# Softmax row sums divided out after the attention product instead of before it, and the q/k load issued in the middle of a pair

## What is computed

```python
def _attn_ref(q, k, v, proj):          # q, k, v: (2, 8, 768, 64); proj: (64, 6)
    q_bits = (einsum('bhsd,dk->bhsk', q, proj) > 0); k_bits = the same of k
    mask = q_bucket[:, :, :, None] == k_bucket[:, :, None, :]     # bucket: the 6 bits as a number
    scores = np.where(mask, scale * (q @ k.T), -1e9)
    scores = scores - max(scores, axis=-1)
    attn = np.exp(scores)
    attn = attn / (np.sum(attn, axis=-1, keepdims=True) + 1e-09)
    return attn @ v                                              # then x: (1536, 512)
def _moe_ref(x):  return ((x @ w1) * (x @ w2)) @ w3 @ w_out      # 512 -> 1024 -> 512
def _moe2_ref(x): return (sigmoid(x @ w_gate) * (x @ w_val)) @ w_out   # 512 -> 1536 -> 512
```

## Time and profile before

| | |
|---|---|
| three runs | 819.89, 815.14, 820.67 us |
| span of the profiled execution, first to last instruction | 813.6 us |
| TensorE busy | 780.8 us (96%) |
| VectorE busy | 385.2 us (47%) |
| ScalarE busy | 381.8 us (47%) |
| GpSimd busy | 232.3 us (29%) |
| attention stage, from the first pair's step 1 to the first MLP matmul | 21.62 to 315.92 us |

### The profile page before, as it was taken

One profiled execution on the slowest core, in us unless ns is written; L12 is line 12 of the kernel. 1 busy time (PEld: TensorE's weight loads), 2 busy tenths in 40 slices (PEclk: granted clock), 3 DMA queues, 4 the chain that ended last, 5 costly groups with the idle time before them and its releaser, 6 DMA issues.

```text
span 813.6 us, 11907 instructions
## 1 busy us (share of the span) xinstructions
PE 780.8 (96%) x3992; PEld 675.8 (83%) x3992; DVE 385.2 (47%) x888; ACT 381.8 (47%) x678; POOL 232.3 (29%) x146
## 2 busy tenths in 40 slices
PE   6799999999799998999999999999999999999998
PEld 4677887879597887999999888888888888888886
DVE  5799999999999996422222111111111111121220
ACT  5688888888688896323322121222313312221211
POOL 3767365462627332211211121113212312100000
PEclk9999999999999999999999999999999999999999
DMA  6662534537343400100000002002202010000101
GB/s 157 195 168 64 148 84 123 123 94 169 77 113 99 118 28 27 52 27 27 26 0 0 1 27 77 27 2 77 77 1 77 14 63 26 0 26 27 39 26 39
DMA packets 22055, 51.68 MB, mean 64 GB/s; under 512 B 3304, under 2 KB 5992, under 8 KB 22032
## 3 DMA queue, kind: packets, MB, share of 16 engines
q1 hardware_dynamic: 21808, 51.32, 22.5%
q10 hardware_dynamic: 224, 0.07, 0.0%
HBM read 29.43 MB, written 3.15 MB: 40 GB/s over the span
## 4 chain that ended last, share of the span: by engine, by line
PE 80%; DVE 7%; SPq 5%; DMA 5%; issue 2%; ACT 1%; DVEq 0%; ACTq 0%
PE pair_bank L930 14%; PE pair_bank L929 14%; PE pair_bank L928 14%; PE bank L930 6%; PE bank L929 6%; PE bank L928 6%; PE bank L853 5%; PE pair_bank L826 5%; DMA qk_raw<-in_qk 5%; PE bank L838 5%; SPq L218 3%; DVE rowmax L648 2%; DVE pt_lo L681 2%; DVE prob L673 2%; SPq L223 1%
## 5 line engine op out<-in xcount | busy, mean ns | idle before, releaser
L360 POOL TENSOR_TENSOR w_lo<-w_raw,w_hi 128x1024 fp32r<-128x1024 f32 (+1 forms) x36 | 69.5, 1931 | 194.1 <-ACT w_hi L445 192.8
L929 PE MATMUL pair_bank<-x_lo,w_hi 128*128 128x512 f32 (+1 forms) x320 | 117.4, 367 | 0.0
L928 PE MATMUL pair_bank<-x_hi,w_hi 128*128 128x512 f32 (+1 forms) x320 | 117.4, 367 | 0.0
L930 PE MATMUL pair_bank<-x_hi,w_lo 128*128 128x512 f32 (+1 forms) x320 | 117.4, 367 | 0.0
L445 ACT ACTIVATE pt_hi<-bank 128x384 fp32r<-128x384 f32 x192 | 84.9, 489 | 39.3 <-PE bank L838 38.7
L681 DVE TENSOR_TENSOR pt_lo<-bank,pt_hi 128x384 fp32r<-128x384 f32 x192 | 97.6, 549 | 11.7 <-ACT pt_hi L445 11.3
L838 PE MATMUL bank<-ident,prob 128*128 128x128 f32 x576 | 83.5, 280 | 15.8 <-DVE pt_lo L681 14.0
L463 ACT ACTIVATE prob<-pair_bank,ebias,escale 128x768 f32<-128x768 f32 x96 | 95.3, 992 | 5.0 <-DVE ebias L659 5.0
L838 PEld LDWEIGHTS bank<-ident,prob 128*128 128x128 f32 x576 | 67.1, 142 | 35.5 <-DVE pt_lo L681 12.8
L648 DVE TENSOR_REDUCE rowmax<-pair_bank 128x1 f32<-128x768 f32 x96 | 91.2, 950 | 4.3 <-PE pair_bank L826 3.5
L826 PE MATMUL pair_bank<-mk,sq 128*128 128x384 f32 x384 | 89.6, 356 | 1.9 <-ACT prob L463 1.9
(11 more groups left out here) (104 smaller groups left out, 1332.3 us busy)
## 6 DMA issues: line engine op xcount, KB each, us to landing
sq<-hl SPq DMA_DIRECT2D x45, 192.0 KB
w_raw<-in_w SPq DMA_DIRECT2D x32, 256.0 KB, 2.7
mk<-hl SPq DMA_DIRECT2D x15, 384.0 KB
qk_raw<-in_qk SPq DMA_DIRECT2D x7, 768.0 KB, 4.3
wo_raw<-in_wo SPq DMA_DIRECT2D x10, 512.0 KB, 4.1
v_raw<-in_v SPq DMA_DIRECT2D x16, 192.0 KB, 3.4
w_raw<-in_wg SPq DMA_DIRECT2D x12, 256.0 KB, 3.3
w_raw<-in_wv SPq DMA_DIRECT2D x12, 256.0 KB, 3.6
```

The costliest lines, as they stand in the source:

```text
L360: pool.tensor_tensor(dst, src, hi, ALU.subtract).then_inc(w_ready[j], 1)
L928: pe.matmul(dst, hi, m_hi, start=start, stop=False)
L929: pe.matmul(dst, hi, m_lo, start=False, stop=False)
L930: return pe.matmul(dst, lo, m_hi, start=False, stop=stop)
```

## The change

`prob` stays unscaled, and nothing lies any more between the exponential and its transposition. The attention output is multiplied by 1/sum after the two halves of `pv_bank` have been added. There the query rows lie along the free axis, so the reciprocals, which VectorE has as a column of 128 partitions by 3, must be laid along a row and repeated on 64 partitions. That is done by two DMAs a unit, `spread_norm`: one writes the 384 values as single 4-byte elements to a row in DRAM, SP waits until they have landed, and the second reads the row back into 64 partitions of `norm_all`. `attention_sum` on GpSimd becomes two operations, an addition and a multiplication that waits for `norm_all`. Epsilon and reciprocal are taken once a unit. `q_codes` is scaled by ScalarE at step 4 and no longer by GpSimd. SP's q/k load of pair p + 2 is issued in the middle of pair p, in front of the head-0 assembly, where before the load of pair p + 1 stood at the start of pair p.

```diff
-NORM_ON_ACT = (2,)
...
+        norm_row = nc.dram_tensor("norm_row", (4, HALF), F32, kind="Internal").ap()
+        x_own = [at(f"x_own{j}", [128, HALF], F32, a + j * 1536) for j in range(2)]; a += 3 * KB
+        norm_all = [at(f"norm_all{j}", [128, HALF], F32, a + j * 1536) for j in range(2)]; a += 3 * KB
...
-            def pair(p, first=False):
-
-                if not first:
-                    load_qk(p + 1, p + 1, 2 * p + 2)
+            def spread_norm(p, u):
+
+                hd, hf = u // 2, u % 2
+                normed, before, after, kept = (4 * p + u + 1, 16 * p, 16 * p + 16, 2 * p - 1 + hf)
...
+                sp.wait_ge(rnorm_done, normed)
+                at_least(sp, norm_loaded[u], before)
+                sp.dma_start(norm_row[u, :].rearrange("(t p) -> p t", p=128),
+                             rnorm[:, UQ * u:UQ * u + UQ],
+                             allow_slow_non_contiguous=True).then_inc(row_loaded[u], 16)
+                sp.wait_ge(row_loaded[u], after)
+                at_least(sp, x_done, kept)
+                sp.dma_start(norm_all[hf][D * hd:D * hd + D, :],
+                             norm_row[u, :].partition_broadcast(D)).then_inc(norm_loaded[u], 16)
+
+            def pair(p, last=False):
+
                 load_w3(p + 1, 0, p + 1)
                 load_v(p + 1, 0, p + 1)
+                spread_norm(p, 0)
+                if not last:
+                    load_qk(p + 2, p + 2, 2 * p + 4)
                 assemble(0, p + 2, STEPS * p + QT)
+                spread_norm(p, 1)
                 load_w3(p + 1, 1, p + 1)
                 load_v(p + 1, 1, p + 1)
+                spread_norm(p, 2)
                 assemble(1, p + 2, STEPS * p + STEPS)
+                spread_norm(p, 3)
...
             load_mlp(w1_d, w2_d, 0, 0, U1)
             load_mlp(w1_d, w2_d, 1, 1, U1)
+            for u in range(4):
+                spread_norm(PAIRS - 1, u)
...
             def attention_sum(p, hf):
 
                 pool.wait_ge(x_kept, 4 * p - 1 + hf)
+                pool.tensor_tensor(x_tmp[hf][:, :], x_tmp[hf][:, :], x_own[hf][:, :], ALU.add).then_inc(x_added, 1)
+                pool.wait_ge(norm_loaded[hf], 16 * p)
+                pool.wait_ge(norm_loaded[2 + hf], 16 * p)
+                pool.wait_ge(x_added, 2 * p - 1 + hf)
                 pool.tensor_tensor(x_f[:, bass.ds(p - 1, 1), HALF * hf:HALF * hf + HALF],
-                                   x_f[:, bass.ds(p - 1, 1), HALF * hf:HALF * hf + HALF],
                                    x_tmp[hf][:, :].rearrange("p (t n) -> p t n", t=1),
-                                   ALU.add).then_inc(x_done, 1)
+                                   norm_all[hf][:, :].rearrange("p (t n) -> p t n", t=1),
+                                   ALU.mult).then_inc(x_done, 1)
...
-                        scale_q_codes(p + 1)
...
+            def scale_q_codes(p):
+
+                act.wait_ge(codes_done, 2 * (p + 1))
+                act.activation(q_codes, codes[0:2 * CODES, :], ACT.Copy, scale=PEN).then_inc(q_codes_done, 1)
...
-                    if k % UQ in NORM_ON_ACT:
-                        act.wait_ge(rnorm_done, s + 1)
-                        act.activation(prob[k % 3][:, :], prob[k % 3][:, :], ACT.Copy,
-                                       scale=rnorm[:, k:k + 1]).then_inc(norm_done[k % UQ], 1)
...
+                    if k == 4 and not last:
+                        scale_q_codes(p + 1)
...
-            def normalise(p, k):
-                dve.wait_ge(rnorm_done, STEPS * p + k + 1)
-                dve.tensor_scalar(prob[k % 3][:, :], prob[k % 3][:, :], rnorm[:, k:k + 1], None,
-                                  ALU.mult).then_inc(norm_done[k % UQ], 1)
+            def inverse(p, u):
+                dve.wait_ge(eps_done, 4 * p + u + 1)
+                at_least(dve, row_loaded[u], 16 * p)
+                cols = slice(UQ * u, UQ * u + UQ)
+                dve.reciprocal(rnorm[:, cols], rowsum_eps[:, cols]).then_inc(rnorm_done, 1)
...
+                dve.tensor_tensor(out, own, x_tmp[hf][rows, :], ALU.add).then_inc(x_added, 1)
+                dve.wait_ge(x_added, added)
+                dve.wait_ge(norm_loaded[hf], 16 * PAIRS)
+                dve.wait_ge(norm_loaded[2 + hf], 16 * PAIRS)
+                dve.tensor_tensor(out, out, norm_all[hf][rows, :], ALU.mult).then_inc(x_done, 1)
...
-                pe.wait_ge(norm_done[k % UQ], 4 * p + k // UQ + 1)
+                pe.wait_ge(exp_done, s + 1)
```

More of the change, by code:

```diff
@@ L153, in build @@
         exp_done, eps_done, rnorm_done = sem("exp_done"), sem("eps_done"), sem("rnorm_done")
-        norm_done = [sem(f"norm_done{j}") for j in range(UQ)]
+        row_loaded = [sem(f"row_loaded{u}") for u in range(4)]
+        norm_loaded = [sem(f"norm_loaded{u}") for u in range(4)]
+        x_added = sem("x_added")
         t_done, pt_hi_done, pt_lo_done = sem("t_done"), sem("pt_hi_done"), sem("pt_lo_done")
@@ L196, in load_qk @@
             def load_qk(p, split, projected):
+                if not isinstance(projected, int):
+                    sp.compute_val(split)
+                    sp.compute_val(projected)
                 at_least(sp, hl_ready, split)
@@ L227, in assemble_q_codes @@
                 cq = CODES * hd
-                sp.dma_start(sq[hd][D:D + CODES, 1, :].bitcast(F32), q_codes[cq:cq + CODES, :]).then_inc(assembled[hd], 16)
+                sp.dma_start(sq[hd][D:D + CODES, 1, :].bitcast(F32), codes[64 + cq:64 + cq + CODES, :]).then_inc(assembled[hd], 16)
             def assemble(hd, pairs, scored):
@@ L274, in _ @@
             load_v(0, 1, 0)
-            pair(0, first=True)
-            with sp.Fori(1, PAIRS - 1) as p:
+            pair(0)
+            with sp.Fori(1, PAIRS - 2) as p:
                 pair(p)
+            pair(PAIRS - 2, last=True)
             load_mlp(w1_d, w2_d, 0, 0, U1)
             load_mlp(w1_d, w2_d, 1, 1, U1)
+            for u in range(4):
+                spread_norm(PAIRS - 1, u)
             with sp.Fori(1, KF // 2) as i:
@@ L307, in rounded @@
                 return pool.tensor_tensor(dst, src, zero.broadcast_to(list(src.shape)), ALU.add)
[L309 to L314, removed]
             def qk_split(p):
@@ L533, in _ @@
             act.activation(sq[0][D:D + CODES, 1, :], codes[0:CODES, :], ACT.Copy, scale=PEN).then_inc(first_parts, 1)
-            act.activation(q_codes[:, :], codes[0:2 * CODES, :], ACT.Copy, scale=PEN).then_inc(q_codes_done, 1)
+            scale_q_codes(0)
             exp(0, 0)
@@ L682, in transposed_lo, with attention_out @@
                                       pt_hi[(k // UQ) % 2][cut].bitcast(F32), ALU.subtract).then_inc(pt_lo_done, 1)
-            def attention_out(rows, hf, src):
+            def attention_out(rows, hf, own, added):
                 cols = slice(HALF * hf, HALF * hf + HALF)
-                dve.tensor_tensor(x_f[rows, PAIRS - 1, cols], src, x_tmp[hf][rows, :], ALU.add).then_inc(x_done, 1)
+                out = x_f[rows, PAIRS - 1, cols]
+                dve.tensor_tensor(out, own, x_tmp[hf][rows, :], ALU.add).then_inc(x_added, 1)
[3 more added lines that the diff above has]
+                dve.tensor_tensor(out, out, norm_all[hf][rows, :], ALU.mult).then_inc(x_done, 1)
             def code_half(p, hf, src=fill_bank):
@@ L705, in pair @@
                         row_max(*nxt)
-                    sum_eps(p, k)
-                    if nxt:
                         exp_scale(*nxt)
-                    inverse(p, k)
-                    if nxt:
                         exp_bias(*nxt)
-                    if k % UQ not in NORM_ON_ACT:
-                        normalise(p, k)
+                    if k % UQ == UQ - 1:
+                        sum_eps(p, k // UQ)
+                        inverse(p, k // UQ)
                     if k > 0:
```

34 lines of the change are left out of this document (15 added, 19 removed).

## The result

The changed kernel takes 957.73 us in the median of 4 runs (955.01 to 959.51), against 819.93 us for the kernel before. The ratio is 1.169, with an interval of 1.164 to 1.173. The prediction was 801 us and faster, with a range up to 816; it was wrong in sign, and its range missed by 142 us.

A forecast was written before the change was run, and what follows sets the result against it. TensorE was taken to bound the stage, with late q/k loads and VectorE-GpSimd holds. Span 813.6 - 21 (waits and slow clock) + 2 (SP's queue) = 794.6 us; median 801 us, range 789 to 816.

The forecast's parts named there:

- The queue of SP: SP's four row writes a pair land in 2.5 us each; SP stays just under TensorE's 34.2 us; 2 us charged.
- SP's cycle: SP's time per pair: own work 15.3 us, four row waits, 6 us behind other traffic; 33.7 us in all.
- Rival 2: Row takes 4.0 us, SP's queue binds at 39.7 us a pair, kernel slower at 835 us; chance 0.13 with milder half.
- Pair 0: First pair, 40.54 us with the slow clock in it, falls to 36.5 us: -4 us.
- The five pairs: Pairs from 62.16 to 246.11 us fall from 183.95 us to 5 x 34.2 = 171.0 us: -13 us.
- The last two and what follows: The last two pairs fall from 69.81 us to 65.8 us: -4 us.
- Rival 3: TensorE's transpositions still wait for low parts; only the load and worst holds go: 808 to 812 us; chance 0.10.
- The q/k load: Issued ahead of the previous pair's head-0 assembly, it removes six TensorE waits of about 1.3 us each.
- The last unit's rows: At the stage's end, the last reciprocals' two DMAs are hidden by other work: 0 us, upper end 2 us.
- rival 1: Row takes 3.0 us, SP's cycle is 35.7 us, 8 us lost instead of 2: 807 us; chance 0.17.
- low parts still at the head of TensorE's waits: Sign in the changed profile's TensorE waits that transpositions still wait for VectorE's low parts, 808 to 812 us.
- no operation of VectorE takes over 1.1 us in the loop: Sign of success in the changed profile: with the scaling gone, nothing VectorE runs in the loop is held at full width.

The follow-up runs named there:

- experiment 6: Changed kernel with the reciprocal row written in 128-byte blocks after a VectorE transposition, and each row's read issued later than its write: 800.71 us, ratio 0.977.
- without rows: Changed kernel without the reciprocal row's DMAs and their waits, norm_all set to ones, so the division is left out: 796.42 us, ratio 0.976.
- blocks alone: Changed kernel with the reciprocals transposed on VectorE and the row written as 128 rows of 128 bytes, nothing else changed: 806.1 us, ratio 0.989.
- experiment 2: Kernel before the change with only the q/k load moved ahead of the head-0 assembly: 808.06 us, ratio 0.991; again 809.05 us, 0.988.
- the version with 8 bytes: Changed kernel with the row's 384 4-byte pieces written 8 bytes apart and the read taking a weight row instead: 839.03 us.
- the control: Changed kernel with the row still written side by side, but the read taking a weight row instead of the reciprocals: 966.11 us.
- experiment 1: Changed kernel with the same DMAs, but other work on SP's queue between each row's write and its read: 819.42 us, ratio 1.005.

## Why the prediction was wrong

**The step that failed** is the landing of the row write in "The queue of SP": 2.5 us, with 2.0 and 4.0 as its ends, from the output store and the smallest load. It measured 9.0. Both neighbours have few or separate pieces; neither writes pieces side by side into the same few hundred bytes, and nothing made the slower of them an upper bound. I said that no row shows such a write, and then let the far end of the range rest on two that were different in just this. The fixed cost of about 2 us that the Trainium skill gives ("DMA: Bandwidth & Descriptors", in the part on the anatomy of a DMA, which treats DMAs issued by GpSimd, where these are SP's), which I put beside it, was right for the same 384 pieces 256 bytes apart (2.1 us) and wrong by 7 us for them side by side.

**The formula behind it has the right lever, but that its sums fit is in part luck.** SP's cycle of 15.3 + 4 x (landing + 0.6) + 6 with seven pairs and 2.4 us of slack gives, with 9.0 us, 7 x (59.7 - 34.2) - 2.4 = 176 us lost against 21 won: a span of 969 against 956.5 measured. With 4.1 us it gives a cycle of 40.1 and a span of 813.6 - 21 + 39 = 832, against 837.2. But a landing is measured from the issue and holds the time behind other traffic already, so the 6 us are counted twice: at 9.0 us a pair is 55.5 us and not 59.7. These 7 x 4.2 = 29 us too much stand against the 22.6 us at the end of the stage, for which the sum has nothing. At 4.1 us the five pairs between 61.85 and 267.45 us do take 41.1 each, but of other things: SP still waits 5 us in each for the query codes, and TensorE for the held epsilon addition. (A slip without weight: the issues of the earlier trace rows go up to 2.03 us; 1.85 is the median.)

**Rival 2 was the case that came**, by its own mechanism: "four round trips in one queue in order, in which each waiting SP holds the assembly behind it". Its break-even of 3.5 us was measured as about 3.1, and its 835 us for a row of 4.0 as 839 for 4.1. It got 0.13 and no part beyond 4 us. The price of one unseen operation decided the sign, at 24 us of time for each us, and such a lever wanted more chance and a longer tail.

**The gains were sized right where nothing was held.** Pair 0: -4 expected, -4.8 in the version of experiment 6 and -5.1 without rows, but +0.2 in the changed kernel and -0.1 on blocks alone. The five pairs: 34.2 us each expected, 34.3 without rows and 34.6 with them, so -13 expected and -12.3 and -10.9 measured. The last two and what follows: -4 expected, -4.5 and -3.6. In sum a span of 794.6 was expected, and 793.8 was measured once the row was fast and out of the way. That is the fastest of six executions; their median time is 800.7 us, and 801 was forecast. VectorE's busy time in a pair fell to 28.9 us without rows, as expected, and to 30.1 with the transpositions. Rival 3 fell with it: in the version of experiment 6 TensorE waits for low parts 5.5 us in all, against 14.0 in the earlier trace rows.

**The q/k load** was counted as a gain of its own, six waits of 1.3 us. Alone it gave 6 us in the five pairs, by another way (experiment 2), and its real part in this change I didn't see: without it the rows hold it back until the end of the pair.

**The last unit's rows** were set at 0 to 2 us, "meanwhile made without them". With landings of 9 us four of them stand one behind the other, and TensorE waited 22.6 us.

**The signs.** SP waiting for almost nothing but the row was named as a sign of rival 1 or 2, and so were scores that wait for an assembly DMA; both were there. But "low parts still at the head of TensorE's waits is rival 3" was a bad sign: they stood at its head, with 87.6 us, and it was SP. A wait for VectorE tells nothing until one knows what VectorE waits for.

**What VectorE can be held on** the forecast had wrong as well. It took from the earlier trace rows that one-column operations are never held, and named as a sign that no operation of VectorE takes over 1.1 us in the loop. But the change makes the epsilon addition three columns wide, and this one was held: 3.32 us in pair 0, 2.07 near the end of the stage, and up to 2.5 in the pairs of the version with 8 bytes. Row maxima and low parts never were (0.96 and 0.56 us at most). The rule of the Trainium skill on the shared port pair ("SBUF — State Buffer", "Who interferes with whom"), which I had applied to the wide operations alone, names tensor-scalar operations among those that can lock GpSimd out and be locked out; the trace agrees, with 3.32 us beside GpSimd's 3.42. On blocks alone it cost pair 0 its gain, some 5 us; in the changed kernel the late rows have a part in that too, since the control, not held there, takes 43.8 us for pair 0. The sign doesn't hang on it.

## What to carry to other kernels

A row in DRAM used to turn a column of partitions into a line costs what its pieces cost to land, and every wait for it in a queue that runs in order costs that time to all that stands behind: write it in pieces of a hundred bytes or so (a small transposition first), and put other issues between the write and the wait for it. Before a load is left behind such a wait, see when the wait can end at the earliest. And where a sum hangs on one operation that no row shows, multiply its price by how often the queue meets it, and give the far side of the range the weight that this product has.

## What the runs showed of the hardware

- 384 writes of 4 bytes: 9.0 us to land side by side in 1.5 KB, 4.1 us at 8 bytes apart, 2.9 at 16, 2.1 at 256. 128 writes of 12 bytes side by side: 2.7 us. 128 writes of 128 bytes: 2.5 us.
- The time isn't spent in moving: from 187 to 193 us of the changed kernel, while SP waits for a write issued at 184.35 that lands near 191.7, the DMA engines are busy 0.00 of the time and move 0 GB/s. The same again behind the write issued at 435.87 us: from 439 to 445 us nothing moves. That the pieces have gone by then and their receipt is awaited is my reading; no view shows it. What takes this long wasn't tried. The small extent of the whole isn't enough for it, since the 128 pieces of 12 bytes fill the same 1.5 KB.
- The same side-by-side write takes 11.1 us in the median when other issues follow it on the queue (experiment 1), and SP then waits at most 7.8 us for it.
- A VectorE tensor-scalar operation of 128x3 values, 0.16 us by itself, takes 3.32 us when a 3.42 us GpSimd subtraction has started 0.13 us before it (3.33 beside 3.42 on blocks alone); the 128x1 form was never over 0.156 us in 96 times.
